# Routing by 224 slots, set-up moved forward, two drains moved forward, and filler products in a two-layer mixture-of-experts kernel

## The reference

```python
# layer 1: only tokens with a positive skip score, each to its best expert
do_compute = x @ w_skip > 0
xc = x[do_compute]
logits = xc @ w_gate
e_idx = np.argmax(logits, axis=1)
probs = np.exp(logits - logits.max(-1, keepdims=True))
probs /= probs.sum(-1, keepdims=True) + 1e-09
for e in range(E):
    mask = e_idx == e
    h = np.maximum(xc[mask] @ w1[e], 0.0)
    y[mask] = gate_w[mask, None] * (h @ w2[e])
out[do_compute] = xc + y

# layer 2: tokens and experts are matched greedily by falling logit,
# at most N // E = 384 tokens for an expert
h = np.maximum(x[mask] @ w1[e], 0.0)
out[mask] = h @ w2[e]
```

## Time and profile before

| | |
|---|---|
| Three runs | 870.97 us median (869.21 to 871.67) |
| Profiled execution | 873.73 us, of which the span of instructions is 871.9 us |
| Mean granted TensorE clock | 0.944 of full speed |
| TensorE busy | 758.9 us, 87% of the span, 5529 matmul records |
| VectorE, ScalarE, GpSimd busy | 538.1, 457.4 and 165.0 us |

### The profile page before, as it was taken

How to read it: one execution, slowest core, us unless ns; L and a number is a source line. 1 busy time by engine, 2 the same in 40 slices (tenths; PEclk the granted TensorE clock), 3 DMA queues, 4 the chain that set the end, 5 groups by cost and what they waited for, 6 DMA issues and landing times. The chain is left out here.

```text
span 871.9 us, 15492 instructions
## 1 busy us (share of the span) xinstructions
PE 758.9 (87%) x5529; PEld 691.1 (79%) x5529; DVE 538.1 (62%) x1441; ACT 457.4 (52%) x919; POOL 165.0 (19%) x186
## 2 busy tenths in 40 slices
PE   0899999999739999999999911899999999999994
PEld 0799999998729998999999801879797888888893
DVE  3977678677467775665666327585756767675320
ACT  2789889888415443554554301535354555535350
POOL 5000000000020222022121121132324141423221
PEclk9999999999959999999999855899999999999998
DMA  8888999998273466345663003658676757769651
GB/s 180 177 196 210 258 211 275 214 266 249 101 244 126 149 218 234 109 150 200 228 212 113 5 10 118 183 175 213 203 190 235 187 189 182 211 176 302 193 110 39
DMA packets 66425, 157.93 MB, mean 181 GB/s; under 512 B 11542, under 2 KB 14998, under 8 KB 66336
## 3 DMA queue, kind: packets, MB, share of 16 engines
q1 hardware_dynamic: 54624, 121.05, 47.3%
q0 software_dynamic: 11712, 35.73, 16.9%
HBM read 119.11 MB, written 23.50 MB: 164 GB/s over the span
## 5 line engine op out<-in xcount | busy, mean ns | idle before, releaser
L1607 PE MATMUL r_ph<-r_xh,r_w1h 128*128 128x384 f32 x256 | 90.8, 355 | 0.0
L557 ACT ACTIVATE pr<-pr,nmx 128x232 f32<-128x232 f32 (+1 forms) x192 | 79.9, 467 | 17.0 <-DVE nmx L653 17.0
L1607 PE MATMUL r_ph<-r_xh,r_w1l 128*128 128x384 f32 x256 | 86.6, 338 | 0.0
L1607 PE MATMUL r_ph<-r_xl,r_w1h 128*128 128x384 f32 x256 | 86.3, 337 | 0.0
L992 PE MATMUL m_ph<-m_xh,m_w1h 128*128 128x256 f32 (+1 forms) x288 | 85.5, 297 | 0.8 <-DVE m_hl L1194 0.7
L1117 ACT ACTIVATE m_hh<-m_ph 128x256 fp32r<-128x256 f32 (+1 forms) x72 | 26.8, 372 | 111.9 <-PE m_ph L992 105.4
L992 PE MATMUL m_ph<-m_xl,m_w1h 128*128 128x256 f32 (+1 forms) x288 | 83.2, 289 | 0.0
L992 PE MATMUL m_ph<-m_xh,m_w1l 128*128 128x256 f32 (+1 forms) x288 | 83.1, 289 | 0.0
L430 PE MATMUL sc<-kk,qh 128*128 128x256 f32 x192 | 58.9, 328 | 23.7 <-DVE ql L631 23.7
L653 DVE CUSTOM_DVE_ANT_0 pr<-sc,bias 128x232 f32<-128x232 f32 (+1 forms) x192 | 64.9, 374 | 19.1 <-PE sc L431 18.6
L1621 PE MATMUL r_py<-r_w2h,r_hh 128*128 128x512 f32 x192 | 76.5, 398 | 0.0
(11 more groups left out here) (272 smaller groups left out, 1954.1 us busy)
## 6 DMA issues: line engine op xcount, KB each, us to landing
r_w<-moe_w SPq DMA_DIRECT2D x64, 512.0 KB, 5.2
m_w<-moe_w SPq DMA_DIRECT2D x36, 512.0 KB, 5.6
row_buf<-moe_w SPq DMA_DIRECT2D x9, 2048.0 KB, 8.7
r_w2l<-r_w POOLq DMA_DIRECT2D x32, 512.0 KB, 5.3
k_raw<-kI SPq DMA_DIRECT2D x32, 416.0 KB, 8.2
q_raw<-qT SPq DMA_DIRECT2D x32, 384.0 KB, 9.4
x_rows<-row_buf SPq DMA_DIRECT2D x8, 1536.0 KB, 8.9
vo<-vL SPq DMA_DIRECT2D x16, 384.0 KB
```

The costliest lines, as they stand in the source:

```text
L557: nc.scalar.activation(pr[n % PRS][:, t, lo:CW], pr[n % PRS][:, t, lo:CW], ACT.Exp, bias=nmx[n % PRS][:, t:t + 1], scale=-1.0).then_inc(ex ...
L1607: last = nc.tensor.matmul(ph[m % 4][:, 0:CAP], w[:, c, m * P:(m + 1) * P], x[:, c, :], start=(c == 0 and a == 0), stop=(c == KC - 1 and a ...
```

## The change

1. **Drains.** GpSimd gets one `g.drain()` in layer 1, behind the z scatter of block 6 and ahead of the row scatter of block 7, and one in layer 2, in the last block ahead of its first scatter. The drains at the ends of the program's blocks stay.
2. **Set-up.** The constants of layer 2 are filled in the attention's block, behind its own; layer 2 no longer waits for `filled`, and its first `bests` reads `logits2` without the masking step.
3. **Marks by expert, table in halves.** `work` and `hot` are laid out expert by token tile, and `picks` is written in two halves, each with its own increment of `tabled`.
4. **A gather ahead.** GpSimd issues an indirect DMA whose row numbers are all out of bounds, before it waits for the list. Each tile of block 0 has its own semaphore.
5. **Tiles turned singly.** `first_turn` turns block 0's first tile when it has landed, then the second, into four PSUM banks, and `h_products` of block 0 waits for the splits of the bank that it overwrites.
6. **Filler products.** 18 products of 128x512 in bfloat16, whose result nobody reads, stand on TensorE before the first transposes of either layer.
7. **224 slots.** A block's second tile has 96 rows: the h products have 224 columns, and transposes, scatters and y products of the second tile work on 96 rows. The overflow block keeps 128 slots.

```diff
+BUSY1, BUSY2 = 18, 18
+ROWS1 = (128, 96)
+WIDE1 = sum(ROWS1)
...
-OVER = N // P - TT1
+OVER = N // P - 1
...
+                for dst, value in ((fullf, 0.0), (pen2, 0.0), (owner, 0.0), (left, float(CAP)), (shut, 0.0)):
+                    keep_link(g.memset(dst[:], value))
...
+            def rows_in(k, t):
+                return ROWS1[t] if isinstance(k, int) and k < E else P
+
             def width(k):
-                return P * len(tiles(k))
+                return sum(rows_in(k, t) for t in tiles(k))
...
-                pool.wait_ge(cleared, 2)
+                g.memset(never[:], NO_ROW).then_inc(cleared, 1)
+                pool.wait_ge(cleared, 3)
                 pool.wait_ge(stored, 32 * B)
+                g.indirect_dma_start(xg[1][:, 0, :], None, x_dram, bass.IndirectOffsetOnAxis(ap=never[:], axis=0),
+                                     bounds_check=N - 1, oob_is_err=False).then_inc(warmed, 16)
                 pool.wait_ge(listed, 1)
                 gather(0, 0)
+                pool.wait_ge(warmed, 16)
...
                 z_scatter(E - 2, 0)
+                g.drain()
                 scatter(E - 1, 1)
...
+                def first_turn():
+
+                    for t in tiles(0):
+                        pe.wait_ge(first_gathered[t], 16)
+                        for c in range(KC):
+                            last = nc.tensor.transpose(turned_to(0, c)[:, t * P:t * P + rows_in(0, t)], xg[0][0:rows_in(0, t), t, c * P:(c + 1) * P],
+                                                       ident[0:rows_in(0, t), 0:rows_in(0, t)])
+                            if t == TT1 - 1:
+                                last.then_inc(x_turned, 1)
...
                 def h_products(k, s, m, W):
+                    if isinstance(k, int) and k == 0 and 0 < m < KC:
+                        pe.wait_ge(x_high, m + 1)
+                        pe.wait_ge(x_low, m + 1)
...
+                def keep_busy(times):
+
+                    for i in range(times):
+                        nc.tensor.matmul(py[0][:], onesb1[:], busy[:, 0:512], start=True, stop=True)
...
                 row_table()
-                turn(0, 0, (0, 1))
-                turn(0, 0, (2, 3))
+                keep_busy(BUSY1)
+                first_turn()
                 for k in range(E - 1):
-                    one_block(k, k % 2, BLK, lambda chunks: turn(k + 1, (k + 1) % 2, chunks))
+                    one_block(k, k % 2, WIDE1, lambda chunks: turn(k + 1, (k + 1) % 2, chunks))
...
-                    v.tensor_tensor(picks[:], grid(low, P), lane_grid[:], ALU.is_equal).then_inc(tabled, 1)
+                    for half in (slice(0, NT // 2), slice(NT // 2, NT)):
+                        v.tensor_tensor(picks[:, :, half], low[:, half].unsqueeze(1).broadcast_to([P, P, NT // 2]),
+                                        lane_grid[:, :, half], ALU.is_equal).then_inc(tabled, 1)
...
                     if k < E - 1:
                         gather(k + 1)
+                    else:
+                        g.drain()
                     for t in range(TT - 1):
                         scatter(k, t)
...
                 table(0)
+                keep_busy(BUSY2)
                 turn(0)
...
-                dve.wait_ge(filled, FILLS)
-                bests()
+                bests(logits2)
```

More of the change, by code:

```diff
@@ L148, in build @@
         rows2 = sb("rows2", [P, E, CAP // P], I32)
+        fullf = sb("fullf", [P, CANDS], BF16)
+        pen2, owner = sb("pen2", [P, NT]), sb("owner", [P, NT])
+        left, shut, alive = (sb(x, [P, E]) for x in ("left", "shut", "alive"))
+        steps_f = sb("steps_f", [P, TRIES, CANDS])
+        after, lane1, onesb = sb("after", [P, P], BF16), sb("lane1", [P, P], BF16), onesb1
+        ids, idsf = sb("ids", [P, NT, 2], BF16), sb("idsf", [P, 2, NT])
+        busy = lane_grid[:].rearrange("p l t -> p (l t)")
         late = ExitStack()
@@ L762, in build @@
             by_expert = [P, E, NT]
-            work = tb("work", shape, BF16)
+            work = tb("work", by_expert, BF16)
             hot = tb("hot", by_expert, BF16)
@@ L851, in _ @@
                 load2(0, 0)
-                sp.wait_ge(gathered[0], moved(0))
+                for t in range(TT1):
+                    sp.wait_ge(first_gathered[t], 16)
                 for k in range(1, E):
@@ L954, in turn @@
                         pe.wait_ge(gated, 1)
-                    pe.wait_ge(gathered[s], moved(k))
+                    pe.wait_ge(gathered[s], gathered_by(k, s))
                     for c in chunks:
@@ L1000, in y_products @@
                     for a, (h, w) in enumerate(((hh, w2h), (hh, w2l), (hl, w2h))):
-                        last = nc.tensor.matmul(py[t % 2][:], h[:, c, t * P:(t + 1) * P], w[:, c, :],
+                        r = rows_in(k, t)
+                        last = nc.tensor.matmul(py[t % 2][0:r, :], h[:, c, t * P:t * P + r], w[:, c, :],
                                                 start=(c == 0 and a == 0), stop=(c == FC - 1 and a == 2))
@@ L1060, in ahead @@
                         turn(E, 0, chunks)
-                one_block(E - 1, 1, BLK, ahead)
+                one_block(E - 1, 1, WIDE1, ahead)
                 with pe.If(n < 1):
@@ L1183, in z_part @@
                             dve.wait_ge(z_scattered[s], moved(k - 2))
-                        T = len(tiles(k))
-                        v.tensor_copy(zo[s][:, 0:T, :], pt[0][:, BLK:BLK + T * E].rearrange("p (t e) -> p t e", e=E)).then_inc(z_kept, 1)
+                        for t in tiles(k):
+                            r = rows_in(k, t)
+                            last = v.tensor_copy(zo[s][0:r, t, :], pt[0][0:r, BLK + t * E:BLK + (t + 1) * E])
+                        last.then_inc(z_kept, 1)
                 def one_block(k, W):
@@ L1397, in build @@
             totals, incl, excl = (tb(x, [P, E, NT]) for x in ("tot", "incl", "excl"))
-            left, shut, need, cnt, alive, value = (tb(x, [P, E]) for x in ("left", "shut", "need", "cnt", "alive", "value"))
+            need, cnt, value = (tb(x, [P, E]) for x in ("need", "cnt", "value"))
             needc = tb("needc", [E, 1])
```

152 lines of the change are left out of this document (74 added, 78 removed).

## The result

The changed kernel takes 847.52 us, the median of four runs (846.0 to 847.98), against 870.68 us for the kernel before in the same comparison: a ratio of 0.973, interval 0.971 to 0.975. It is faster by 2.7%. Forecast were 842 us with a range of 836 to 853.

The account below looks back on a forecast made before the run. TensorE was taken to bound the kernel between layer 1's blocks, nearly always busy at full clock, with the routings as exceptions; terms summed to 28.9 us, from 873.73 to 844.8 profiled, 842 us median, range 836 to 853.

Parts of the forecast that it names:

- Drains: GpSimd's drains at layer 1's and the kernel's end: 83 ns per DMA since the last drain; gain 10.0 us.
- Set-up: Start of layer 2: the search's first reduction no longer waits for GpSimd's constants or a masking step; gain 2.8 us.
- First routing until the rows landed: Layer 1's routing up to the gathered rows: (a) to (c) together bring the last row 3.15 us earlier.
- (a): First routing, marking steps: laid out by expert, the last writes in a line; gain 0.5 us, bounds 0 and 0.7.
- (b): First routing, table in halves: half of TensorE's products lies beside the second half; gain 0.85 us.
- (c): First routing, first two gathers: a dummy gather takes the first-time cost ahead; gain 1.8 us, bounds 0 and 2.
- the port: Rival on block 0's gathers: the port, not the first time, made them long; without the 1.8 us, 844; chance 0.09.
- From the rows to the first y product: Block 0's start: 4.1 us gained, 2.2 by clock, 1.2 by turning, 0.7 by narrower products counted elsewhere.
- 224 columns: h products of eight layer 1 blocks: a step takes 112 ns instead of 120; gain 6.3 us.
- the slow form: Rival: under 256 columns products leave their fast form, 196 ns a step, 58 us more, 906 us; chance 0.06.
- Second routing: Layer 2's first twelve products: at full clock they end with the last low part; gain 2.4 us, bounds 0 and 2.9.
- the clock falls in more places: Rival: four more stretches at half clock, costing 1.7 us each; 849 us; chance 0.04.

Follow-up runs that it names:

- the splits held: Changed kernel with VectorE's low parts of block 0's weights held until GpSimd has issued both gathers of block 0; 853.1 us, one run.
- the kernel again: The changed kernel itself, unaltered, run beside the last group on the same chip; 849.39 us (847.7 to 851.6), ratio to before 0.974.

## Why the prediction was right, and where it was off

- **Drains: 10.0 forecast, 9.98 measured** in the profiles, 10.1 by taking them out. The five drains at ends, 3, 6, 51, 52 and 80 DMAs, lie on 82 ns for each and 50 more. The records of the early ones last 5.9 and 8.9 us, not 3.8 and 6.4, but they begin while DMA instructions ahead are still at work. From the end of the last of these the drain of layer 1 takes 457.06 - 453.22 = 3.8 us for its 46 DMAs, which is the price; that of layer 2 takes 827.70 - 819.65 = 8.05 for its 77, 1.7 more than the price. So what was off is the term for the second drain, and it stayed within the gap all the same. The margin there was smaller than I wrote: the drain ended at 827.7 and the scatter began at 829.8.
- **Set-up: 2.8 forecast, 2.64 measured** (5.68 us to 3.04 from the layer's first row to the search's first reduction). The size was right and its reason half right, so the size owes something to luck: 1.1 is the move, 0.4 the masking step, about 1.2 the three fills fewer, which the forecast did not count.
- **First routing until the rows landed: 3.15 forecast, 1.87 measured** (19.62 to 17.75 us). (a) gave -0.2 instead of 0.5: the step that failed is that I weighed the layouts and not what runs beside them. GpSimd's fill was in the trace, and one of the steps, begun a little later against it, waited for the second fill; with it held the gain is the forecast 0.5. (b) gave 0.76 for 0.85. (c) gave 0.93 for 1.8: I let the first-time cost explain both long gathers. For the second the rival was right that the splits make it long; the port that it is named after stands untested. The gather in layer 2 that I held against it shows only that not every gather beside a split is long; the same holds for the first one here, 1.10 us, and for the third with the splits held, 1.29. What decides between them stays open. The other 0.4 us, unforecast, lie in the pauses around the gathers.
- **From the rows to the first y product: 4.1 forecast (3.4 + 0.7), 4.01 measured.** The clock came back at 252.2, after about 12 slow fillers, and the run without them puts 2.4 us on it, where 2.2 was forecast.
- **224 columns: 112 ns forecast, 111.6 measured**; the slow form, 0.06, did not come. The gate products gave 0.21 us a block, the upper bound of 1.7 us and not the 0.8 taken. An undisturbed block fell from 26.02 to 24.95 us. Over seven blocks that would be 7.5 us, but block 0's first y product to block 7's end gave 6.35. Nearly 0.9 of the rest went to waits: those of TensorE's within the blocks are the 1.1 and 0.5 us above, where the group of before has 0.8 in all (columns: busy us, mean ns, idle us ahead and what ended it):

```profile
L992 PE MATMUL m_ph<-m_xh,m_w1h 128*128 128x256 f32 (+1 forms) x288 | 85.5, 297 | 0.8 <-DVE m_hl L1194 0.7
```

- **Second routing: 2.4 forecast, 1.93 measured.** The clock was full, and the products then waited for the low parts, the last at 529.54 + 1.94 = 531.48.
- **The sum: 28.9 forecast, 27.7 measured** for the pair of profiles. So 1.2 of the 5.5 us by which 842 was too low come from the terms.
- **The other 4.3 us are the step from the profile to the median.** I took 0.997 for both kernels. The profile of before was 2.8 us above its median, that of the changed kernel 1.5 below its own. Behind it stands the rival "the clock falls in more places", which I gave 0.04 and thought of as steady. It happens in part of the executions: 3.4 us of half clock in blocks 0 to 3 in one profile, 16.9 in another. Four more stretches would give 849, the rival said; the kernel again, with that much more in its profile, had a median of 849.4.

## What to carry to other kernels

A GpSimd queue that has issued many DMAs makes the drain at a block's end long, here 82 ns for each; a drain set into a gap ahead takes that off the end. When TensorE has become the bound, look for its small waits: here one of 1.1 us was followed in six of ten profiles by stretches at half clock, and holding the fills and moving some 6.5 us of VectorE's work into its pauses beat the changed kernel by 3.8 to 5.6 us. Before a gain is booked to an instruction's shape or its place, look at what the engines beside it do at that moment, and weigh the term by an execution whose clock you have compared with the others.

## What I had not expected of the hardware

- **The floor of a float32 step ends late.** 128, 224 and 240 columns take 111.7, 111.6 and 111.8 ns, 256 take 119.8. The Trainium skill, "TensorE: Matmul & The Clock Gate", section "Back-to-back issue gap", has N/2.4 plus a constant for a matmul by itself, and says that with a load of weights for each one this counts too little where N is small; with the constant that 256 columns give, 13.1 ns, 240 would take 113.1 and 224 would take 106.4. The trace agrees with the warning and not with the formula: at 224 columns it is 5 ns short, and the prediction, which quoted the formula alone, was right to go by the rows. The floor lies near the 107 ns for a load of weights in its section "LDWEIGHTS (loading the stationary operand)". It moves with the clock: at 1.2 GHz steps of 128, 224, 240 and 256 columns all take 213 ns.
- **A drain with DMAs in flight can last longer** than 82 ns for each and 50 more. Past the end of the last DMA instruction it takes 3.8 us with 46 DMAs and 2.1 with 23 in layer 1, where the price is 3.8 and 1.9; in layer 2 it takes 8.1 with 77, 6.4 with 37 and 4.0 with 40 (in the middle), where the price is 6.4, 3.1 and 3.3. Ahead of those with 77 and 37 the last DMA lands 5.7 us after its instruction begins. All these drains end 1.0 to 3.2 us after the last landing. How waiting for it and clearing the others overlap was not tried.
- **A fill of GpSimd's can hold a tiny step of VectorE's.** 24 numbers took 0.94 us instead of 0.18, by when the step began against the fill.
- **The same program differs by up to 5.6 us** with how long the granted clock is at its lower level, 3.4 or 17 us over blocks 0 to 3. One of the falls comes in six of ten profiles behind a wait of 1.1 us, and in none without it.
